# The packed product of two heads at a time: 64 weight columns and 128 moving columns instead of 32 and 64

## What is computed

```python
def _attn_ref(q, k, v, p):                   # 8 batches, 8 heads, 576 rows, 64 columns; p has 32 rows
    p_packed = sm_attn(p, k, v)              # softmax(scale * p @ k.T) @ v
    return sm_attn(q, p_packed, p_packed)
# x = the 8 heads side by side, 512 columns
gate = sigmoid(causal convolution of x, 5 taps)
x = (gate * (x @ w_val)) @ w_out
h = relu(x @ w_in); u, v = halves of h
v_s = w_spatial @ layernorm(v) + b_spatial
out = (u * v_s) @ w_final
```

## Time and profile before

| what | value |
|---|---|
| median of 3 runs | 563.41 us (561.39 to 564.57) |
| profiled execution | 564.57 us, its span 562.8 us |
| TensorE busy | 548.4 us, 97% |
| VectorE busy | 448.9 us, 80% |
| ScalarE busy | 315.2 us, 56% |
| mean granted TensorE clock | 0.99 of full |

### The profile page before, as it was taken

One profiled execution on the slowest core, in us unless ns is written; L12 is line 12 of the kernel. 1 busy time (PEld: TensorE's weight loads), 2 busy tenths in 40 slices (PEclk: granted clock), 3 DMA queues, 4 the chain that ended last, 5 costly groups with the idle time before them and its releaser, 6 DMA issues.

```text
span 562.8 us, 12566 instructions
## 1 busy us (share of the span) xinstructions
PE 548.4 (97%) x5072; PEld 377.1 (67%) x5072; DVE 448.9 (80%) x846; ACT 315.2 (56%) x499; POOL 10.3 (2%) x16
## 2 busy tenths in 40 slices
PE   6899899999999999999999999999999999999997
PEld 4345458775777658775677658775677658774785
DVE  2599899996988878895988879895988869894740
ACT  3179676655647644765547644666547645663522
POOL 0000000000000000000000000000000000000000
PEclk9899799999999999999999999999999999999999
DMA  8990810016200540016200450015300200011002
GB/s 274 286 343 6 257 77 1 2 42 218 84 2 1 168 172 0 0 42 204 95 0 0 151 189 0 0 42 175 124 0 0 84 0 0 0 42 43 1 1 84
DMA packets 24134, 45.15 MB, mean 80 GB/s; under 512 B 2033, under 2 KB 11249, under 8 KB 23090
## 3 DMA queue, kind: packets, MB, share of 16 engines
q1 hardware_dynamic: 19506, 35.42, 19.5%
q10 hardware_dynamic: 4608, 9.44, 4.5%
HBM read 35.42 MB, written 9.44 MB: 80 GB/s over the span
## 4 chain that ended last, share of the span: by engine, by line
PE 90%; DMA 3%; DVE 3%; ACT 2%; SPq 1%; issue 1%; DVEq 0%
PE X L472 20%; PE X L448 17%; PE X L488 17%; PE X L429 15%; PE Y L407 7%; DMA wval_sb<-w_val 3%; PE Y L330 2%; PE Y L393 2%; PE X L434 2%; DVE gate L800 2%; PE Y L298 2%; PE Y L346 1%; PE X L496 1%; PE Y L359 1%; PE Y L311 1%
## 5 line engine op out<-in xcount | busy, mean ns | idle before, releaser
L800 DVE SCALAR_TENSOR_TENSOR gate<-xT,conv_sb,gate 128x576 f32<-128x576 f32 x128 | 94.7, 812 | 0.3 <-ACT gate L1135 0.3
L488 PE MATMUL X<-late,wfin_h 128*128 128x288 f16 x512 | 83.8, 286 | 0.3 <-DVE late L700 0.3
L472 PE MATMUL X<-wsp_h,vn_h 128*128 128x288 f16 x320 | 65.4, 286 | 0.0
L488 PEld LDWEIGHTS X<-late,wfin_h 128*128 128x128 f16 x512 | 49.2, 98 | 14.8 <-issue 1.7
L448 PE MATMUL X<-gvT_h,wfused_h 128*128 128x288 f16 x256 | 52.3, 286 | 0.0
L488 PE MATMUL X<-late,wfin_l 128*128 128x288 f16 x256 | 52.3, 286 | 0.0
L472 PE MATMUL X<-wsp_h,late 128*128 128x288 f16 x256 | 52.3, 286 | 0.0
L448 PE MATMUL X<-gvT_h,wfused_l 128*128 128x288 f16 x256 | 52.3, 286 | 0.0
L472 PE MATMUL X<-wsp_l,vn_h 128*128 128x288 f16 x256 | 52.3, 286 | 0.0
L448 PE MATMUL X<-gvT_l,wfused_h 128*128 128x288 f16 x256 | 52.3, 286 | 0.0
L429 PE MATMUL X<-wfused_h,gvT_h 128*128 128x512 f16 x128 | 49.2, 384 | 0.8 <-ACT u_res L1135 0.8
(11 more groups left out here) (163 smaller groups left out, 1070.5 us busy)
## 6 DMA issues: line engine op xcount, KB each, us to landing
k_sb<-kT SPq DMA_DIRECT2D x16, 576.0 KB, 5.2
q_sb<-qT SPq DMA_DIRECT2D x8, 1152.0 KB, 6.2
outT<-u_res ACTq DMA_DIRECT2D x32, 288.0 KB, 2.1
v_sb<-v_rows SPq DMA_DIRECT2D x8, 1024.0 KB, 5.3
late<-w_spT SPq DMA_DIRECT2D x1, 1152.0 KB
stage_a<-w_outT SPq DMA_DIRECT2D x4, 256.0 KB, 12.7
stage_b<-w_in SPq DMA_DIRECT2D x4, 256.0 KB, 13.2
v_sb<-v_rows SPq DMA_DIRECT2D x8, 128.0 KB, 5.5
```

The costliest lines, as they stand in the source:

```text
L472: last = mm(X[1 - c % 2][:, a, 0:HALF], x, w[:, a * HALF:(a + 1) * HALF], start=i == 0, stop=i == len(terms) - 1)
L488: last = mm(X[1 - c % 2][:, a, 0:HALF], w[:, d, c * P:(c + 1) * P], x[:, d, a * HALF:(a + 1) * HALF], start=d == 0 and i == 0, stop=d == C ...
L800: tap = nc.vector.scalar_tensor_tensor(gate[:, j, :], xT[:, j, k:k + S], conv_sb[:, j, k:k + 1], gate[:, j, :], ALU.mult, ALU.add)
```

## The change

In the packed product two heads are taken together. The loop over four heads becomes one over two pairs r: the weights are 64 columns of exp1T (both heads' queries), the moving operand the 128 columns of v of both heads, the output 64 partitions x 128 columns of Y[0][:, u, 0:128]. Of each pair's output the blocks where queries of one head meet v of the other are not wanted. The masked copy on VectorE reads the 128 columns as they stand and multiplies by the same mask, which puts zero there. `packed` holds what it held before. Waits, semaphores, the order of everything and the other matmuls stay.

```diff
@@ packed_product
                     k = P if t < FULL else TAIL
-                    for h in range(PAIRS):
-                        head = slice((PAIRS * u + h) * HP, (PAIRS * u + h + 1) * HP)
-                        packs = slice(NP * h, NP * (h + 1))
-                        last = mm(Y[0][packs, u, 0:HP], exp1T[0:k, u, t, packs], v_sb[0:k, t, head],
-                                  start=t == 0, stop=t == ST - 1)
+                    for r in range(2):
+                        j = 2 * u + r
+                        last = mm(Y[0][64 * r:64 * r + 64, u, 0:P], exp1T[0:k, u, t, 64 * r:64 * r + 64],
+                                  v_sb[0:k, t, j * P:(j + 1) * P], start=t == 0, stop=t == ST - 1)
@@ pack
-                nc.vector.scalar_tensor_tensor(packed[:, u, :].rearrange("p (r c) -> p r c", r=2),
-                                               Y[0][:, u, 0:HP].unsqueeze(1).to_broadcast([P, 2, HP]),
-                                               rsum1[:, u:u + 1],
-                                               head_mask[:, :].rearrange("p (r c) -> p r c", r=2),
-                                               ALU.mult, ALU.mult).then_inc(packed_ready, 1)
+                nc.vector.scalar_tensor_tensor(packed[:, u, :], Y[0][:, u, 0:P], rsum1[:, u:u + 1],
+                                               head_mask[:, :], ALU.mult, ALU.mult).then_inc(packed_ready, 1)
```

## The result

The changed kernel takes 569.82 us (median of 4 runs, 569.39 to 571.42), the kernel before 562.72 (4 runs with the one beside it, 561.39 to 564.57). The ratio is 1.0128, with a 95% interval of 1.0105 to 1.0150: slower by 7.1 us (by the interval 5.9 to 8.4). Forecast were 570.3 us and a ratio of 1.012. Over all 31 runs of the changed kernel on record and all 32 of the kernel before, those beside the experiments too, the medians are 569.94 and 562.54 us, 7.4 apart.

A forecast was written before the change was run, and what follows sets the result against it. TensorE, busy 97% of the span, was taken to bound the kernel. Six steady batches at 0.96 us gave 5.8, batch 1 added 1.1 and batch 0 nothing: 6.9 us, from 563.41 to 570.3 us, range 568.0 to 573.2.

The forecast's parts named there:

- TensorE sets the time, gap or no gap: Whole kernel: TensorE busy 97% of the span; every nanosecond the packed product gains or loses counts where TensorE runs without gaps.
- A step is moving columns, two clocks each, side by side in strips: Packed product: 128 moving columns take 0.107 us a step, two records side by side, still ten steps a unit.
- The unit, 1.34 to 1.37 us: One of a batch's two packed-product units: ten steps plus 0.27 to 0.30 us for fill and shape changes, up from 0.83.
- The wait for exp1T goes: Between the two packed-product units: the longer first unit removes the second's 0.08 us wait for ScalarE's copies.
- The covers behind it: After the packed product: six v matmuls, 1.40 us, still hide VectorE's chain before the packed transpose, within 0.05 us.
- Batch 0 is hidden: First batch: its extra 1.0 us disappears in TensorE's 1.82 us gap before L346, waiting for w_val; nothing added.
- Batch 1, 1.1 us: Second batch, at 1.2 GHz: packed product +2.1 us, the clock's return giving some back; likeliest +1.1, up to +2.1.
- The six v matmuls of batch 1 at about 1.3 us: Behind batch 1's packed product: predicted sign, 1.3 to 1.4 us instead of 2.40, as the full clock returns.
- Cost by instructions: Packed product: rival that fewer records save time, 0.56 us a batch visit, giving 558.9 us; chance 0.05.
- No overlap: Packed product: rival that the two 64-column strips run one after the other, +3.1 us a visit, giving 586; chance 0.04.
- Hidden time: Steady iteration: rival that something other than TensorE sets the pace and a wait absorbs the loss, near 564.5; chance 0.05.
- the fourth: Rival: packed product grows as forecast, but a cover breaks or the half clock lasts longer, 573 to 577; chance 0.08.

The follow-up runs named there:

- the padded and later one: Kernel before with the 64-row last tile zero-filled to 128 rows and the packed product moved half a v tile later; 560.04 us, ratio 0.9963.
- one strip at a time: Changed kernel with its two loops exchanged, all five row tiles of one head pair before the other's; 589.08 us in one run.
- the padded wide kernel: Changed kernel with the packed product's 64-row last tile multiplied as 128 rows, the upper 64 zero; 566.42 us, ratio 1.0059.
- the second profile of before: Kernel before, unchanged, profiled once more for the clock around 60 us and the w_val load; 563.14 us in one run.
- the narrow moving operand: Changed kernel with 64 weight columns but only 64 moving columns, first head of each pair, and the old masked copy; 564.0 us, ratio 1.0024.

## Why the prediction was right, point by point

**TensorE sets the time, gap or no gap.** Right. The visit grew by 1.04 us and the iteration by 1.04; in the other kernels with visits from 1.61 to 5.51 us the two go together within 0.01 us as well. Where they don't (visit -0.49, iteration -0.40, the padded and later one) the difference is at the packed transpose.

**A step is moving columns, two clocks each, side by side in strips.** Right, and now shown apart: changing the columns alone brings 1.79 or 2.73 us, whatever the weights. The step is 0.109 us where I had 0.107.

**The unit, 1.34 to 1.37 us.** Slightly small. It is 1.39 (2.78 a visit, forecast 2.68 to 2.74). Most of the miss is in the step: ten steps of 0.109 and not of 0.107 us are 0.05 more a visit. What is left of a unit, the fill and two changes of shape, is 0.30, the upper end of the 0.27 to 0.30 that I had. Its parts are not those of the row it was taken from: in the tail of v, in fp16, the second pair starts 0.13 us after the first, with fp32 weights of 64 columns 0.16 us. So 6 x 0.96 = 5.8 should have been 6 x 1.04 = 6.2.

**The wait for exp1T goes.** Right: the visit is one piece in the chain.

**The covers behind it.** Right. VectorE's chain and the packed transpose as the changed kernel's timeline has them:

```profile
199.21 0.35 DVE L713 SCALAR_TENSOR_TENSOR packed<-Y,rsum,head_mask 128x128 f32<-128x128 f32 x1
199.60 0.29 DVE L719 TENSOR_TENSOR packed_pair<-packed 128x128 f32<-128x128 f32 x1
...
200.02 0.27 PE L298 MATMUL Y<-ident,packed_pair 128*128 128x128 f32 x1
```

The pair sum ends at 199.89 and the transpose starts at 200.02, 1.31 us after the v tile's first matmul at 198.71, as before (199.10 and 200.40). The copy takes its old 0.35.

**Batch 0 is hidden.** Right as far as the profile goes: the visit there is longer by 1.1 us and TensorE still waits for the w_val load before L345:

```profile
14.30 2.85 PE L329 MATMUL Y<-v_sb,exp1T 128*64 128x128 f32 x40 [0.39 <-ACT exp1T L1131]
...
23.80 1.09 PE L345 MATMUL Y<-wval_sb,packedT 64*32 64x512 f32 x16 [0.59 <-DMA wval_sb<-w_val]
```

The gap is 0.59 us where it was 1.82, but that difference is no measure of the cover. The visit began 0.72 us later, the load landed 0.96 us earlier, and in the first profile of before TensorE was at the low clock from 15.5 to 18.9 us, so that four records of L496 took 3.55 us behind the visit, where they take 1.98 in the changed kernel. With the same matmuls and the old masked copy the gap is 1.74. Timelines of before and of that kernel:

```profile
15.24 3.55 PE L496 MATMUL X<-stage_b,stage_a 128*128 128x512 f32 x4
...
24.56 1.09 PE L345 MATMUL Y<-wval_sb,packedT 64*32 64x512 f32 x16 [1.74 <-DMA wval_sb<-w_val]
```

How much cover is left goes with where the loads fall; it was used up only with one strip at a time, whose visit there is 5.58 us long and which has no gap before L345.

**Batch 1, 1.1 us.** The size was right, +1.1 by the comparison above, the reason was not, and that is luck: I took the stretch at 1.2 GHz for a trait of that place in the kernel, put 2.1 us on the visit for it, and took 1.0 off again for the clock coming back. The stretch falls differently from run to run in both kernels. Had I gone by the full clock, the term would have been one more 1.04. In one run the case that I had described can be seen: in the padded wide kernel the clock is low from 63.0 to 66.4 us, the visit of batch 1 takes 4.04 us for 2.33, and the six v matmuls behind it 1.40. By the same error the profiled execution was forecast at 571.5 us and took 568.32: the first profile of before has two low stretches, from 15.5 to 18.9 and from 59.9 to 66.7 us, where the changed kernel's profile has the full clock. The six v matmuls of batch 1 at about 1.3 us, named as a sign of being right, are no sign either: they take 1.40 in the second profile of before too.

Together: 6.2 + 1.1 = 7.3 us. Measured are 7.1, and 7.4 over all runs. The forecast 6.9 is small by the 0.4 of the steady visits, less than the runs can tell. That 570.3 and 569.82 stand so close has a part of chance: the forecast started from 563.41, the median of three runs, and the kernel before measured 562.72 beside the change.

**The rivals.** Cost by instructions fell with the narrow moving operand (half the records, 1.79 us and not 1.2). That kernel should also have gained by the floor of about 25 ns from start to start that the Trainium skill gives ("TensorE: Matmul & The Clock Gate", Back-to-back issue gap), since it halves the starts; the runs do not agree: 80 starts at 25 ns would be 2.0 us, the visit of before takes 1.75, and for matmuls in different strips the starts stand 0.007 us apart. For the change the prediction took this floor wrongly. It is for up to 64 moving columns; for 128, which the changed kernel has, the same section of the Trainium skill gives 134 cycles, at 2.4 GHz an estimate of 0.056 us. Twenty of these are 1.1 us a unit against forty floors of 1.0, so the section promised no gain. Measured, such a record on fp32 takes 0.109 us in its strip, and two strips share it. No overlap fell with the strips taken one at a time. Hidden time fell with the iteration. Of the fourth, no cover broke.

## What to carry over

When small matmuls stand side by side in column strips of the array, count steps: moving columns times clocks per column, and only matmuls in different strips share a step. Joining two narrow matmuls into one of twice the width and twice the columns halves the instructions, but doubles each step (0.056 to 0.109 us here) and leaves their number; here what it adds is masked away, so it lost. On a core whose TensorE has no gaps, look at changes of shape as well: filling up a 64-row tail with zeros saved about 0.13 us for each change that went.

## What the runs showed that I had not expected

- A change of the array's shape (128 to 64 rows, or on to other matmuls) costs 0.13 to 0.14 us in the narrow form (0.90 less 0.77 us for one; 1.74 less 1.25, less the 0.08 of waiting, for three) and 0.15 in the wide one (2.78 less 2.33 us, for three), the longer first step behind it included, and zeros in place of the missing rows are cheaper than changing. By this alone the kernel before could be made 0.2% faster, and 0.4% with the units put where their inputs are ready.
- The first step after a change of shape is longer than the steps behind it, by an amount that goes with the weights and not with the moving columns: 0.024 us with 32 columns of fp32 (0.080 for 0.056 with 64 moving columns, 0.133 for 0.109 with 128) and 0.05 with 64 columns (0.107 for 0.058, 0.160 for 0.109). Within a stream none of this shows.
- The stretches at 1.2 GHz in the prologue differ from run to run of one kernel: in the two profiles of the kernel before, from 59.9 to 66.7 us and from 60.85 to 64.20; the first has one more from 15.5 to 18.9, where the second has the full clock, and the second one from 23.4 to 26.8. Two spans of single profiles could so differ by 3.7 us where the medians differ by 7.1. What decides where they fall was not tried.
